# Token routing of a mixture of experts behind attention: gather in place of scatter, and expert windows written out without jumps

## What is computed

```
def _attn_ref(q, k, v, centroids):            # q, k, v: (2, 8, 768, 64), 16 centroids
    mask = q_assign[:, :, :, None] == k_assign[:, :, None, :]     # nearest centroids
    scores = np.where(mask, scale * q @ k.T, -1e9)
    return softmax(scores) @ v

def _moe_ref(x, expert_emb, tau, w1, w2):     # x: (1536, 512), 8 experts
    logits = xn @ en.T / tau                  # rows of x and of expert_emb normalized
    expert_idx = np.argmax(logits, axis=1)
    gate_w = softmax(logits)[np.arange(N), expert_idx]
    for e in range(E):                        # w1[e]: (512, 1024), w2[e]: (1024, 512)
        mask = expert_idx == e
        h = np.maximum(x[mask] @ w1[e], 0.0)
        out[mask] = gate_w[mask, None] * (h @ w2[e])

def _moe2_ref(x, w_a, w_b, w_out):            # (512, 1536), (512, 1536), (1536, 512)
    return (x @ w_a) * (x @ w_b) @ w_out
```

## Time and profile before

| | before |
|---|---|
| median of 3 runs | 898.36 us (896.52 to 900.96) |
| the profiled execution's own time | 907.04 us |
| its span | 905.2 us |
| TensorE busy | 829.7 us, 92% |
| VectorE busy | 419.8 us, 46% |
| ScalarE busy | 289.8 us, 32% |
| GpSimd busy | 108.2 us, 12% |
| mean granted TensorE clock | 0.934 |

### The profile page before, as it was taken

The page is one execution under the profiler, slowest core; times in us unless marked ns, Lnnn a source line. Parts: engine busy times, 40 slices in busy tenths (PEclk is TensorE's granted clock), DMA queues, the critical chain, the costliest instruction groups (busy, mean ns, idle before and its releaser), DMA issues.

```text
span 905.2 us, 13586 instructions
## 1 busy us (share of the span) xinstructions
PE 829.7 (92%) x5377; PEld 744.9 (82%) x5378; DVE 419.8 (46%) x676; ACT 289.8 (32%) x499; POOL 108.2 (12%) x116
## 2 busy tenths in 40 slices
PE   5699999999999999229899999989999999999996
PEld 4499999999999897129899999878888888888885
DVE  5746776677766532705355555453413211131111
ACT  3123333333333235405345455444312111121111
POOL 6002221122112010470000000000000100010001
PEclk9559999999999789659899999999999999999998
DMA  5213333333223123573555566551000100010001
GB/s 132 53 40 81 97 79 78 80 99 98 77 64 81 34 94 107 180 198 119 191 182 207 198 209 206 173 185 47 1 1 0 47 1 1 0 47 1 1 1 46
DMA packets 61661, 80.06 MB, mean 88 GB/s; under 512 B 17992, under 2 KB 38696, under 8 KB 61600
## 3 DMA queue, kind: packets, MB, share of 16 engines
q1 hardware_dynamic: 59296, 72.90, 26.8%
q0 software_dynamic: 2304, 6.31, 1.9%
HBM read 57.11 MB, written 14.17 MB: 79 GB/s over the span
## 4 chain that ended last, share of the span: by engine, by line
PE 89%; issue 5%; DVE 3%; DMA 1%; ACT 1%; SPq 0%; POOLq 0%; POOL 0%; ACTq 0%; DVEq 0%
PE bank L1191 14%; PE bank L1383 7%; PE bank L1384 7%; PE bank L1385 7%; PE pair L1149 5%; PE pair L1338 3%; PE pair L1340 3%; PE pair L1339 3%; PE first_pair L1175 3%; PE first_pair L1177 3%; PE bank L1126 2%; PE bank L1122 2%; PE first_pair L1326 2%; PE first_pair L1400 2%; PE first_pair L1402 2%
## 5 line engine op out<-in xcount | busy, mean ns | idle before, releaser
L1191 PE MATMUL bank<-v_sb,prob 128*128 128x66 f32 x1152 | 149.1, 282 | 0.0
L1191 PEld LDWEIGHTS bank<-v_sb,prob 128*128 128x128 f32 x1152 | 148.8, 203 | 0.1
L827 DVE TENSOR_REDUCE neg_max<-pair 128x1 f32<-128x768 f32 x93 | 88.7, 954 | 72.6 <-PE pair L1149 72.6
L1383 PE MATMUL bank<-x_hi,wt 128*128 128x512 f32 x288 | 112.7, 391 | 2.9 <-DVE x_lo L1060 2.9
L1384 PE MATMUL bank<-x_lo,wt 128*128 128x512 f32 x288 | 112.8, 392 | 0.0
L1385 PE MATMUL bank<-x_hi,wt 128*128 128x512 f32 x288 | 112.7, 391 | 0.0
L1079 DVE TENSOR_TENSOR g_sb<-bank,a_sb 128x512 f32<-128x512 f32 x36 | 24.9, 692 | 176.6 <-PE bank L1385 175.0
L573 ACT ACTIVATE prob<-first_pair 128x384 f32<-128x384 f32 x128 | 59.7, 489 | 134.9 <-PE first_pair L1177 133.9
L947 DVE TENSOR_TENSOR wt<-w_raw,wt 128x2048 fp32r<-128x2048 f32 x41 | 93.7, 2288 | 16.8 <-ACT wt L640 16.7
L640 ACT ACTIVATE wt<-w_raw 128x2048 fp32r<-128x2048 f32 x41 | 78.0, 1908 | 0.0
L1338 PE MATMUL pair<-ht_hi,wt 128*128 128x240 f32 x256 | 71.2, 278 | 0.0
(11 more groups left out here) (212 smaller groups left out, 1585.5 us busy)
## 6 DMA issues: line engine op xcount, KB each, us to landing
w_raw<-in_moe_w_dram SPq DMA_DIRECT2D x32, 1024.0 KB, 5.2
x_slots<-out_sb SPq DMA_DIRECT2D x15, 512.0 KB, 3.7
q_raw<-in_q_dram SPq DMA_DIRECT2D x16, 192.0 KB, 2.4
k_raw<-in_k_dram SPq DMA_DIRECT2D x16, 192.0 KB, 2.5
v_sb<-in_v_dram SPq DMA_DIRECT2D x16, 192.0 KB, 3.1
qb<-qa SPq DMA_DIRECT2D x16, 192.0 KB, 2.6
kc<-kd SPq DMA_DIRECT2D x16, 192.0 KB, 2.9
w_raw<-in_moe_w_a_dram SPq DMA_DIRECT2D x3, 1024.0 KB, 5.2
```

The lines of the kernel that those rows point to most:

```text
L827: dve.tensor_reduce(neg_max[n % 2][:, t:t + 1], masked_in(n, t)[:, :, 0:HALF], AX.XY, ALU.max, negate=True).then_inc(mx_done, 1)
L1191: last = pe.matmul(o_tiles[:, t, :], prob[s][:, j, t * P:(t + 1) * P], v_in_sb[u][:, j, :], start=(j == 0 and t == 0), stop=(j == NT - 1), ...
L1383: pe.matmul(to[:, :], w[0], x2_hi[:, kk, :], start=(kk == 0), stop=False)
```

## The change

- **Logits.** In the last two rounds all 12 tiles are turned, one at each of six places of a round, tiles 6 to 11 without their last 128 columns (heads 14 and 15 write those). The logits are made tile by tile, token-major: `x_t` is the stationary operand and the 8 columns of `en_t` move. After the last head, the last 128 columns of six tiles are turned and added. `tau` is folded into `en_t`; the pick reads logits that are not yet divided by the row's norm; the norm comes later (`shift_logits`).
- **Token list.** No x scatter. VectorE compares each token's place with the starts of 28 half windows of 120 lanes (`ge`); GpSimd multiplies by the high and the low part of the token number (`ge_tok`); 12 bf16 matmuls against a one-hot of the lane sum that to a list of tokens per lane and half window (`tok_of`). The rows of x go in token order to DRAM (`x_rows`) by three plain stores: the first batch in round 9, the rest around the last two heads. GpSimd gathers each half window by an indirect DMA. The zero writes are gone.
- **Experts.** Eight windows are written out; a loop of pairs after them is entered only if there are more than eight. Each window, not each expert, has weights loaded by a table of experts. The first expert's first chunk is loaded in round 9 and split in round 14; the second expert's four chunks are loaded once the tables are there. The low parts of chunks 2 and 3 and the gates (`gates`, and so `meta_ready`) move from before the first window into VectorE's program of that window.

```diff
         def early_tile(r, place):
-            return [NT - 3 * (HEADS - r) + place] if HEADS - 2 <= r < HEADS else []
+            return [NT * (r - HEADS + 2) + place] if HEADS - 2 <= r < HEADS else []
+        def early_parts(j):
+            return KD if j < NT else KD - 1
...
+        def windows(eng, more, window):
+            for g in range(E):
+                window(g, g % 2)
+            with eng.If(more):
+                with eng.Fori(0, more) as i:
+                    for par in range(2):
+                        window(2 * i + E + par, par)
...
-                if 1 <= r <= X_ZEROS:
...
-                    sp.dma_start(rows, zeros[:, None, :].to_broadcast([P, 2, DM])).then_inc(zeroed, 16)
+                if r == H + 1:
+                    sp.wait_ge(x_done, H)
+                    store_rows(0, 0, DM)
+                    load_expert(0, 0, 0, (0,))
+            sp.wait_ge(x_done, HEADS - 2)
+            store_rows(1, 0, DM - 2 * D)
             sp.wait_ge(x_done, HEADS)
+            store_rows(1, DM - 2 * D, DM)
             sp.wait_ge(t1_free, len(t1_index))
+            load_expert(0, 0, 0, (1, 2, 3))
+            sp.wait_ge(tables_ready, 1)
...
-            pool.wait_ge(slots_ready, 1)
-            pool.wait_ge(zeroed, 16 * X_ZEROS)
-            pool.wait_ge(x_done, HEADS)
-            for j in range(TT):
-                pool.indirect_dma_start(x_slots[:, :], bass.IndirectOffsetOnAxis(ap=slot_of[:, j:j + 1], axis=0),
-                                        x_tok[:, j, :], None).then_inc(scattered, 16)
+            pool.wait_ge(ge_ready, 1)
+            for part in range(2):
+                last = pool.tensor_tensor(ge_tok[:, :, part, :], ge[:],
+                                          tok_parts[:, part, :, None].to_broadcast([P, TT, TILES + 1]), ALU.mult)
+            last.then_inc(ge_tok_ready, 1)
+            def gather(g):
+                for i in range(2):
+                    if g > 0:
+                        pool.wait_ge(sx_full, 2 * g)
+                    index = tok_of[0:WT, 2 * g + i:2 * g + i + 1]
+                    pool.indirect_dma_start(x_slot[i][0:WT, :], None, x_rows[:, :],
+                                            bass.IndirectOffsetOnAxis(ap=index, axis=0)).then_inc(x_in[i], 16)
+            pool.wait_ge(tok_ready, 1)
+            pool.wait_ge(x_stored, 48)
+            gather(0)
+            gather(1)
             pool.wait_ge(meta_ready, 1)
             for j in range(TT):
                 pool.indirect_dma_start(meta_rows[:, :], bass.IndirectOffsetOnAxis(ap=y_pos[:, j:j + 1], axis=0),
                                         meta[:, j, :], None).then_inc(meta_out, 16)
+            pool.wait_ge(tables_ready, 1)
+            more = more_pairs(pool)
+            for g in range(2, E + 1):
+                gather(g)
...
+            def logits(j):
+                pe.wait_ge(xt_taken, j + 1)
+                for kk in range(early_parts(j)):
+                    last = pe.matmul(pair[:, 1, j * E:(j + 1) * E], x_t[j % 2][:, kk, :], en_t[:, kk, :],
+                                     start=(j == 0 and kk == 0), stop=(kk == KD - 1), skip_group_check=True)
+                last.then_inc(lg_done, 1)
+            def early(r, place):
+                for t in early_tile(r, place):
+                    turn_x(t)
+                    if t >= 1: logits(t - 1)
...
+            for j in range(TT):
+                if j % NT == 0:
+                    pe.wait_ge(lanes_ready, j // NT + 1)
+                last = pe.matmul(bank[2][0:WT, 0:2 * (TILES + 1)], at_lane[:, j, :],
+                                 ge_tok[:, j, :, :].rearrange("p a c -> p (a c)"), start=(j == 0), stop=(j == TT - 1))
+            last.then_inc(tok_full, 1)
...
+            def window(g, par):
                 ht_low(g, 0)
+                if isinstance(g, int) and g == 0:
+                    low_chunk(0, 2, 2)
                 ht_low(g, 1)
+                if isinstance(g, int) and g == 0:
+                    low_chunk(0, 3, 3)
+                low_chunk(g + 1, 0, 4 * (1 - par))
                 ht_low(g, 2)
                 ht_low(g, 3)
+                low_chunk(g + 1, 1, 4 * (1 - par) + 1)
                 x_low(g + 1)
+                if isinstance(g, int) and g == 0:
+                    gates()
+                low_chunk(g + 1, 2, 4 * (1 - par) + 2)
+                low_chunk(g + 1, 3, 4 * (1 - par) + 3)
```

More of the change, by code:

```diff
@@ L118, in build @@
         out_sb = [sb(f"out_sb{i}", [P, DM], F32) for i in range(2)]
-        zeros = out_sb[0]
         w_raw = []
@@ L468, in _, with refill @@
-            sp.wait_ge(slots_ready, 1)
-            experts(sp, expert)
+            load_expert(0, 0, 0, (1, 2, 3))
+            sp.wait_ge(tables_ready, 1)
+            def refill(n, par, done):
+                e = from_table(sp, 1, n, E - 1)
+                if isinstance(n, int) and n < 2:
+                    load_expert(n, par, e, range(4))
+                    return
+                sp.wait_ge(h_full, HB * done)
+                load_expert(n, par, e, (0, 1))
+                sp.wait_ge(y_full, 2 * done)
+                load_expert(n, par, e, (2, 3))
@@ L470, in _ @@
+            for n in range(1, 4):
+                refill(n, n % 2, n - 1)
             sp.wait_ge(meta_out, 16 * TT)
             sp.dma_start(meta_back[:], meta_rows.rearrange("(j p) c -> p j c", p=P)).then_inc(meta_in, 16)
-            load_chunk(E + 2, 0, 8)
+            for n in range(4, E):
+                refill(n, n % 2, n - 1)
+            more = more_pairs(sp)
+            with sp.If(more):
+                with sp.Fori(0, more) as i:
+                    for par in range(2):
+                        done, n = 2 * i + E - 1 + par, 2 * i + E + par
+                        sp.to_reg(n)
+                        refill(n, par, done)
@@ L473, in _ @@
+            for m, (kind, grp) in enumerate(FF_CHUNKS):
+                done, n, c = 2 * more + E - 1 + m // 4, 2 * more + E + m // 4, m % 4
+                sp.to_reg(n)
+                if m < 8:
+                    if c == 0:
+                        sp.wait_ge(h_full, HB * done)
+                    elif c == 2:
+                        sp.wait_ge(y_full, 2 * done)
+                load_chunk(n, c, m, ff_source(kind, grp), 4)
             for i in range(2):
```

557 lines of the change are left out of this document (289 added, 268 removed).

## The result

| | before | after |
|---|---|---|
| median of the runs | 899.41 us (896.52 to 900.96, 4 runs) | **886.46 us** (884.71 to 890.35, 4 runs) |
| the profiled execution's own time | 907.04 us | 890.35 us |
| its span | 905.2 us | 888.3 us |

The ratio is 0.9866, 95% interval 0.9823 to 0.9908: 12.9 us by the medians, 1.3% or 12.0 us by the ratio. The forecast was 24.2 us and 874. In what follows medians are over all executions of a kernel, and ratios leave out those that ran over 1.5% longer than its fastest.

The account below looks back on a forecast made before the run. TensorE was taken to bound attention, with 52.4 us of mostly idle routing and 195.4 us of experts behind it. Heads +10.2, routing -30.4, experts -13, gather 2 +9: -24.2 from 898.4 gives 874 us, range 862 to 889.

Parts of the forecast that it names:

- Gather 2 behind the scatters: Second window: TensorE idles 6.7 us for gather 2, issued after twelve scatters, plus 2 of low clock; +9 us.
- The routing: Last attention product to first expert matmul: 22 us in place of 52.4; -30.4 us.
- The store of round 9: SyncE's queue in attention: new stores costed at nothing, as transfers end about 7 us before next mask rows; 9 without cover.
- heads 14 and 15: Last two attention heads: 18 more turns, 2.0 us, and 39 logits matmuls, 8.2 us, all on TensorE; +10.2 us.
- experts without jumps: Eight expert windows written out: waits at jumps, the clock behind them and a slow first window go; -13 us.
- Rival 3: Expert windows: instructions come late for want of supply, not for jumps, so the 13 us stay; 887 us, chance 0.15.
- Rival 1: Second window: no wait at gather 2, so the 9 us go; 865 us, chance 0.22.
- GpSimd beside the low part: Second window's scatters: four that meet VectorE's low parts take 1.1 us more each; 4.6 us.
- Six turns, a copy, nine matmuls and the hand-overs: 2.6: Routing, after the last fill at 2.4 us: last turns and logits take 2.6 us, to 5.0.
- the step that named GpSimd's products as the last input: Routing's token list: GpSimd's two multiplies of 348 elements take 1.9 us, to 11.9, before the twelve small matmuls.
- Rival 2: First window starves for second-expert weights asked for late, beside gathers; some 7 us, 881 us, chance 0.15.
- Rival 4: Expert windows: every gather comes late and six windows wait; 42 us, 916 us, chance 0.05.

Follow-up runs that it names:

- idle turns: Idle TensorE products put into the routing's waits of the changed kernel with gather 2 first, scatters two by two, store in three pieces; 864.8 us, ratio 0.9622.
- no jumps: The kernel before with its eight experts written out, without loop, conditional jumps and reads of `bases`; 884.88 us, ratio 0.9888.
- gather first: The changed kernel with gather 2 issued ahead of the twelve scatters on GpSimd; 871.0 us, ratio 0.971.
- store cut: The changed kernel with round 9's store cut into three over rounds 9 to 11, first weight chunk moved to round 12; 884.39 us, ratio 0.9854.
- the pair: The changed kernel with gather 2 ahead of the scatters, store cut in three against store whole, on one chip; 869.11 against 873.88 us.
- idle work: The changed kernel with its scatters behind the last gather and 28 linked memsets in their old place ahead of gather 2; 884.8 us, ratio 0.9901.
- gather-first's second run: The changed kernel with gather 2 ahead of the scatters and the store whole, run again; 873.88 us, ratio 0.9797.
- gather-first with the cut store: The changed kernel with gather 2 ahead of the scatters and round 9's store cut in three; 869.11 us, ratio 0.9744.

## Why the prediction was right in its signs and wrong in its size

Three terms of the sum failed. Gather 2 behind the scatters was put at +9 and cost 15.2, because its landing was priced at 2.7 us and took 10.6. The routing was put at -30.4 and gave -27.0, because TensorE's work in it was priced at full clock, the lane's one-hots were left out and the gathers landed later. The store of round 9 was put at nothing and cost 2 to 5.

| term | forecast | profile of after | the run that isolates it |
|---|---|---|---|
| heads 14 and 15 | +10.2 | +8.8; 10.3 at equal clock | none |
| routing | -30.4 | -27.0 | idle turns: 1.9 of it is clock |
| experts without jumps | -13 | -13.2 (without the second window's excess) | no jumps: -12.9 |
| gather 2 behind the scatters | +9 | +15.2 | gather first: -15.5 |
| store of round 9 | 0 | +5.3 | store cut: 4.8 in the pair; alone 1.1 to 3.4, not told from 0 |

**Heads, right.** 0.21 us for a logits matmul of 8 columns: as with 66 columns, so the columns don't set it, and the loads that the prediction named fit. It was paid in full, as the earlier trace rows had said. No run took the logits away, so the term rests on the trace alone.

**Experts, right.** The jumps cost what the earlier trace rows let expect. Rival 3, in which the waits stay, falls by two kernels: the change and the kernel before without jumps. (The one wait for "issue" of 4.2 us in after stands behind ScalarE's late copy, not at a window's start.) No run parts the jumps from the reads of `bases` that went with them. The rule of the Trainium skill ("Runtime: NRT & Kernel Launch", "Instruction fetch mechanics"), that a taken branch whose target is outside the fetched pages stalls until it is fetched, fits this: -12.9 us for writing the experts out, with all else as it was.

**Gather 2, the step that failed most.** Mechanism, place and issue time were right: `meta_ready` came 20.5 us behind the first expert matmul (20.4 forecast), the second half was issued at 41.2 (41.4). What failed is "an indirect DMA of 256 KB lands 2.7 us after issue": that row was of a lone transfer at the program's end. Of the miss of 6 us, 5.8 is the difference between idle work and scatters ahead of the gather. Even after idle work the landing is 5.3 us and not 2.7. That idle work costs 9.4, so near the forecast's 9, is luck in part: there the gather lands 46.2 us behind the first expert matmul and not 44.1, but TensorE also comes for it later, at 38.9 and not 37.4. Rival 1 (no wait) is refuted; taking the wait away gives 871, where it said 865, and wins 15 us and not 9.

**GpSimd beside the low part, right.** Three scatters took 2.79, 1.86 and 2.08 us in place of 0.96, 3.9 us in all (4.6 forecast), beside VectorE's low parts. That `tensor_tensor` operations leave the writing of descriptors alone, as the Trainium skill has it ("SBUF — State Buffer", "Who interferes with whom"), this trace again does not bear out. (That section also names `tensor_scalar` beside copies and casts among the operations that can contend, which the prediction left out.)

**Routing, 3.4 us short.** The list of tokens was due 13.8 us behind the last product and came at 16.5. About 1.6 of that is TensorE at the lower clock in turns and logits, which the step "Six turns, a copy, nine matmuls and the hand-overs: 2.6" had priced at full clock, though the 1.8 us wait ahead of them was in the reckoning. Another 0.8 is `at_lane`, two one-hots of 720 elements on VectorE, 2.25 us together, which the step that named GpSimd's products as the last input had left out of the chain; 0.2 is a later end of the last fill. The rest, 0.7, is a difference of larger pieces: the second gather was issued 1.8 us behind the list and not 1.3, and landed in 4.7 us and not 2.7, while from landing to first matmul were 2.4 us and not 3.5, and 0.7 had been allowed for collisions. So the landing time was too short here as well, and was mostly made up by chance.

**Round 9, costed at nothing.** The text named the cover (7 us of transfer end before the next mask rows) and the price without it (9). The cover was too thin: the DMA engines were full until 249 us and the copy came 1.94 us late. The profile shows 5.3 us, and the paired runs 4.8; the second profile of gather-first has the same 2 us wait without the low clock, and the cut store alone is not told from after.

**The other rivals.** Rival 2: no weight is awaited in window 0, which loses only its low clock. Rival 4: windows from 2 on are 22.38 us; gather 4, for one, is issued at 463.15 and lands in 5.4 us, 14 us ahead of its turn at 482.95.

The misses add to 6.2 + 3.4 + 2 to 5 = 12 to 15, where forecast and median differ by 11.3; the rest is, by my reading and not shown, the variation of attention between executions. What stays open: why ScalarE's copies come late at the scatters' end, behind waits of 2.0 to 4.6 us where 0.3 and 2.1 are usual. They show in four profiles (after, gather-first's second run, gather-first with the cut store, and idle work, which has its scatters and these waits in the last window), and not in three others with twelve scatters in a row. The releaser is named only as "remote". In gather-first's second run they made one window 3.1 us longer; in after their wait lies within the 15.2, and the cut store alone has the same excess without them.

## What to carry to other kernels

Take the landing time of a transfer from a row with the same neighbours in its queue, not from a lone one: a gather behind twelve tiny scatters took up to 10.6 us where 5.0 is the median and 2.7 was the row at hand. When a queue serves both an urgent and a lazy transfer, put the urgent one first: one moved line was worth 14 to 15.5 us, more than the whole change had brought. And a wait of TensorE of about 2 us can have two prices, itself and the half clock behind it; independent idle products in the waits of the routing gave it back in part, 3.3 us in the profile.

## What the runs showed of the hardware that was not expected

- In after an indirect gather of 120 rows landed 3.5 to 7.8 us after its issue, median 5.0. Right behind twelve scatters of 8-byte rows its second half took 9.1 to 10.6 us in five profiles (after, the cut store alone, gather-first twice and with the cut store), and 5.3 us at the same place in the program behind idle work.
- Float32 products of a 128x128 stationary operand with 8 columns take 0.21 us at the granted clock 1.00, the same as with 66 columns, and 0.45 us (2.73 us for twelve records) at 0.50.
- Idle turns of TensorE in its waits kept the granted clock at 0.76 to 1.00 in stretches of 5 us between 355 and 385 us, where it was 0.50 from 364 to 385 us in after; every real product behind them still had a wait of its own, so they delayed none.
- The half clock doesn't follow every wait: behind 1.94 us near 252 us of after the clock was 0.58, behind 2.03 us at the same place in the second run of gather-first 1.00, and behind 1.99 us in its first run 0.59.
- Twelve scatters issued in one run were followed in four of seven profiles by late copies of ScalarE, behind waits of 2.0 to 4.6 us that name no releaser on the core.
